# One core, a three-stage kernel: block 0's upper channels moved to ScalarE and GpSimd, ten spare matmuls at the head, and new orders for the first 30 tiles

## The reference

```python
w = exp(weight - max) / (sum + 1e-9)          # 8 heads x 7 taps
x = causal 7-tap convolution of x along S     # one tap set per head of 24 channels
# stage 2, 192 -> 2048 -> 192
h = x @ w_in ;  x = (h * clip(h + 3, 0, 6) / 6) @ w_out
# stage 3, its own weights, rational activation
h = x @ w_in
P = a0 + a1*h + a2*h^2 + a3*h^3 ;  Q = 1 + |b0|*|h| + |b1|*h^2
x = (P / (Q + 1e-6)) @ w_out
```

## Time and profile before

| | us |
|---|---|
| median of 3 runs (1224.21 to 1225.36) | 1225.18 |
| profiled execution | 1226.22 |
| its span, first to last instruction | 1224.4 |
| TensorE busy, 5120 matmuls | 1181.0 (96%) |
| ScalarE busy | 1170.0 (96%) |
| VectorE busy | 1165.9 (95%) |
| GpSimd busy | 1068.5 (87%) |

### The profile page before, as it was taken

How to read it: one execution, slowest core, us unless ns; L and a number is a source line. 1 busy time by engine, 2 the same in 40 slices (tenths; PEclk the granted TensorE clock), 3 DMA queues, 4 the chain that set the end, 5 groups by cost and what they waited for, 6 DMA issues and landing times.

```text
span 1224.4 us, 18261 instructions
## 1 busy us (share of the span) xinstructions
PE 1181.0 (96%) x5120; PEld 962.9 (79%) x5120; DVE 1165.9 (95%) x1792; ACT 1170.0 (96%) x2225; POOL 1068.5 (87%) x828
## 2 busy tenths in 40 slices
PE   4989999999999999999999999999999999999976
PEld 3768888888888888888888888888888888888754
DVE  6879999999999999999999999999999999998897
ACT  5779999999999999999999999999999999999996
POOL 5859989899898999989998998989989899998774
PEclk9999999999999999999999999999999999999998
DMA  4400000000000000010000000000000000000000
GB/s 146 147 1 9 1 23 1 23 9 1 23 1 23 10 23 1 1 31 1 22 1 14 18 1 23 1 23 10 1 23 1 23 1 14 1 1 14 1 14 13
DMA packets 10022, 21.17 MB, mean 17 GB/s; under 512 B 1601, under 2 KB 1857, under 8 KB 9921
## 3 DMA queue, kind: packets, MB, share of 16 engines
q1 hardware_dynamic: 9776, 19.56, 5.4%
q10 hardware_dynamic: 144, 0.46, 0.1%
HBM read 13.72 MB, written 6.29 MB: 16 GB/s over the span
## 4 chain that ended last, share of the span: by engine, by line
PE 83%; DVE 7%; ACT 6%; issue 3%; DMA 0%; POOLq 0%; POOL 0%; ACTq 0%; SPq 0%; DVEq 0%
PE h L263 41%; PE y0b_acc L280 5%; PE y0b_acc L281 4%; PE y0a_acc L275 4%; PE y0a_acc L277 4%; PE y0a_acc L276 4%; PE y1a_acc L275 4%; PE y1a_acc L276 4%; PE y1b_acc L281 4%; PE y1a_acc L277 4%; PE y1b_acc L280 4%; ACT num L353 1%; ACT g_hi L445 1%; ACT rsq L394 1%; DVE num L375 1%
## 5 line engine op out<-in xcount | busy, mean ns | idle before, releaser
L390 POOL TENSOR_TENSOR den<-den,sqr 128x512 f32<-128x512 f32 x248 | 359.8, 1451 | 103.7 <-ACT den L364 103.7
L439 POOL TENSOR_TENSOR g_lo<-g,g_hi 128x512 fp32r<-128x512 f32 x255 | 331.1, 1298 | 3.6 <-ACT g_hi L445 3.6
L346 POOL TENSOR_TENSOR g_lo<-r,g_hi 128x512 fp32r<-128x512 f32 x235 | 308.7, 1313 | 4.2 <-DVE g_lo L346 1.6
L380 DVE SCALAR_TENSOR_TENSOR num<-num,coef,h 128x512 f32<-128x512 f32 x256 | 191.5, 748 | 9.1
L375 DVE TENSOR_TENSOR num<-num,h 128x512 f32<-128x512 f32 x256 | 174.9, 683 | 11.9 <-ACT num L353 5.8
L353 ACT ACTIVATE num<-h,coef 128x512 f32<-128x512 f32 x256 | 181.6, 709 | 0.2
L417 DVE SCALAR_TENSOR_TENSOR h<-num,coef,h 128x512 f32<-128x512 f32 x240 | 179.7, 749 | 0.2
L445 ACT ACTIVATE g_hi<-g 128x512 fp32r<-128x512 f32 x256 | 166.5, 650 | 10.7 <-DVE g L424 2.6
L332 DVE SCALAR_TENSOR_TENSOR r<-r,h 128x512 f32<-128x512 f32 x235 | 160.8, 684 | 8.8 <-ACT r L325 8.0
L394 ACT ACTIVATE rsq<-den 128x512 f32<-128x512 f32 x248 | 158.7, 640 | 7.7 <-POOL den L390 5.0
L410 DVE SCALAR_TENSOR_TENSOR den<-den,h 128x512 f32<-128x512 f32 x240 | 163.2, 680 | 1.1 <-ACT h L406 0.7
(11 more groups left out here) (109 smaller groups left out, 2931.8 us busy)
## 6 DMA issues: line engine op xcount, KB each, us to landing
stage_w<-w_pack SPq DMA_DIRECT2D x15, 448.0 KB, 3.3
raw_a<-x_a SPq DMA_DIRECT2D x16, 259.0 KB, 3.5
out<-y_a SPq DMA_DIRECT2D x16, 256.0 KB, 2.8
out<-y_b SPq DMA_DIRECT2D x16, 128.0 KB, 2.4
...
stage_w<-w_pack ACTq DMA_DIRECT2D x1, 448.0 KB, 3.5
...
tap_ab<-taps SPq DMA_DIRECT2D x1, 7.0 KB, 2.9
```

Source lines behind the costliest of these rows:

```text
L346: eng.tensor_tensor(g1_lo[t % 2][:, :], gated(t)[:, :], f32(g1_hi[t % 2][:, :]), ALU.subtract).then_inc(S["g1lo"], 1)
L380: eng.scalar_tensor_tensor(out=n, in0=n, scalar=a1, in1=h2_of(t), op0=ALU.add, op1=ALU.mult).then_inc(S["num1"], 1)
L390: eng.tensor_tensor(den_of(t), den_of(t), sqr[t % 2][:, :], ALU.add).then_inc(S["den_sum"], 1)
L439: eng.tensor_tensor(g2_lo[t % 2][:, :], g2[t % 2][:, :], f32(g2_hi[t % 2][:, :]), ALU.subtract).then_inc(S["g2lo"], 1)
```

## The change

- **Setup.** The taps and coefs are loaded by ScalarE's queue, raw_a and then chunk 0 by SP's. Abs, Sqrt and its table load come before `w_in_hi(0)`. The second half of the taps is scaled on ScalarE.
- **Block 0's b part.** ScalarE makes seven products (256 wide) in the SBUF tiles num and den, GpSimd adds them in six steps into conv_b. `w_in_lo(1)` moves from GpSimd to VectorE, ahead of `cs_b_lo(0)`.
- **Root.** Its steps stand one by one between the taps of `conv_a`; the register loads move from the setup to pass 3.
- **TensorE** starts with ten matmuls of chunk 0 by itself into a bank that nobody reads then.
- **Plans.** START for passes 0 to 10, a new BEGIN for 11 to 19, RAMP for 20 to 29; MIDDLE from 30 (its only edit takes out an entry that is empty there), END unchanged. W_PACE 1.55. `run` keeps one list of placed steps by block, and `cs_b_hi(0)`, `cs_b_lo(0)` are excluded by it.

```diff
+START = {
+    "sync": [("load_a", AHEAD, 0), ("load_b", PAIR_AHEAD, 9, 0), ("load_w", -4)],
+    "tensor": [("in1", 0), ("out1", 4)],
+    "scalar": [("g1hi", 1), ("w_out_hi", 2), ("w_in_hi", 2), ("relu1", -1), ("conv_a_first", AHEAD, -2),
+             ("registers", 3)],
+    "vector": [("conv_b1", AHEAD, (2, 2, 2, 5, 5, 6, 7), 1), ("gate1", 0),
+             ("conv_a", AHEAD, (1, 5, 5, 7, 8, 11)), ("g1lo", 1)],
+    "gpsimd": [("w_out_lo", 1), ("w_in_lo", 1)],
+}
 BEGIN = {
...
-    "scalar": [("relu1", 0), ("y1a_out", SUM1, 0), ("x2b_hi", SUM1, 0), ("conv_b_first", PAIR_AHEAD, 13, 0),
-             ("g1hi", 1), ("cs_b_hi", AHEAD, 16, 0), ("w_in_hi", 0), ("x2a_hi", SUM1, 0), ("w_out_hi", 1),
-             ("cs_a_hi", AHEAD, 10), ("conv_a_first", AHEAD, 1), ("cs_b_hi", AHEAD, 9, 1)],
...
+    "scalar": [("x2a_hi", SUM1, 1), ("conv_b_first", PAIR_AHEAD, 14, 0), ("cs_b_hi", AHEAD, 3, 1),
+             ("x2b_hi", SUM1, 0), ("relu1", 0), ("y1a_out", SUM1, 0), ("g1hi", 1), ("w_out_hi", 1),
+             ("w_in_hi", 1), ("cs_a_hi", AHEAD, 7)],
+    "vector": [("conv_b_head", PAIR_AHEAD, (16, 17, 17), 0), ("conv_a", AHEAD, (4, 4, 4, 7, 5, 7)),
+             ("gate1", 0), ("g1lo", 1), ("x2b_res", SUM1, -1), ("x2b_lo", SUM1, -1), ("cs_b_lo", AHEAD, -9, 1)],
+    "gpsimd": [("w_out_lo", 2), ("cs_a_lo", AHEAD, 14), ("w_in_lo", 2)],
+}
+RAMP = {
...
+    "tensor": [("in2", 0), ("in1", 0), ("out1", 2), ("out2", 4)],
+    "scalar": [("conv_a_first", AHEAD, -1), ("cs_a_hi", AHEAD, 10), ("w_in_hi", 1), ("rsq2", 1), ("relu1", 0),
+             ("rec2", 1), ("abs2", 0), ("w_out_hi", -2), ("sq2", 0), ("lin2", 0), ("g2hi", 2), ("g1hi", 0)],
+    "vector": [("num2", 1), ("conv_b_tail", AHEAD, (10, 11, 12), 0), ("conv_a", AHEAD, (1, 4, 4, 5, 7, 8)),
+             ("g1lo", 2), ("num1", 1), ("g_neg", 2), ("gate1", 0), ("newton", 1), ("g_first", 1)],
+    "gpsimd": [("x2a_lo", SUM1, -3), ("den_sum", 0), ("w_in_lo", -1), ("w_out_lo", 6), ("g1lo", 0), ("g2lo", 2),
+             ("cs_a_lo", AHEAD, 13)],
 }
-W_PACE = 1.35
+W_PACE = 1.55
+START_END, RAMP_END, END_AT = 11, 30, 258
+WARM = 10
...
+        def product_b(eng, j):
+            if j == 0:
+                eng.wait_ge(d_raw_b0, 32)
+                eng.wait_ge(S["setup_s"], 5)
+            scaled(eng, products[j], raw_b[:, j:j + HALF], tap[1][:, j:j + 1]).then_inc(S["product_b"], 1)
+
+        def add_b(eng, j):
+            eng.wait_ge(S["product_b"], j + 1)
+            if j > 1:
+                eng.wait_ge(S["conv_b_tap"], j)
+            first = products[0] if j == 1 else sums_b(0)
+            eng.tensor_tensor(sums_b(0), first, products[j], ALU.add).then_inc(S["conv_b_tap"], 2 if j == 1 else 1)
...
         @block.tensor
+            eng.wait_ge(S["wi_hi"], 1)
+            for _ in range(WARM):
+                eng.matmul(h1_of(H_BANKS - 1), win_hi[0][:, 0:P], win_hi[0][:, 0:BLK], start=True, stop=True)
...
         @block.scalar
-            load_w(eng, 0)
+            eng.dma_start(tap_ab[:, :], taps[:, :]).then_inc(d_tap, 16)
+            eng.dma_start(coef[:, :], coefs[:, :]).then_inc(d_const, 16)
...
-            w_in_hi(eng, 0)
...
+            w_in_hi(eng, 0)
+            eng.wait_ge(S["setup_v"], TAPS_READY)
+            scaled(eng, tap[1], tap[1], tap_sum[:, 1:2]).then_inc(S["setup_s"], 1)
+            for j in range(K):
+                product_b(eng, j)
+            cs_a_hi(eng, 0)
             w_in_hi(eng, 1)
+            cs_b_hi(eng, 0)
             w_out_hi(eng, 0)
-            cs_a_hi(eng, 0)
...
         @block.vector
             for j in range(K):
                 conv_a_tap(eng, 0, j)
+                if j < 2:
+                    normalize(1, j)
+                else:
+                    eng.wait_ge(*((S["setup_s"], 4) if j == 2 else (S["setup_v"], n_own[0])))
+                    own(refine[j - 2]())
+            eng.wait_ge(S["setup_v"], n_own[0])
+            eng.tensor_tensor(b1_root, s, t, ALU.subtract).then_inc(S["root_done"], 1)
             cs_a_lo(eng, 0)
-            for j in range(K):
-                conv_b_tap(eng, 0, j)
+            w_in_lo(eng, 1)
+            cs_b_lo(eng, 0)
...
         @block.gpsimd
             w_in_lo(eng, 0)
-            w_in_lo(eng, 1)
+            for j in range(1, K):
+                add_b(eng, j)
             w_out_lo(eng, 0)
```

More of the change, by code:

```diff
@@ L36 @@
     "tensor": [("in1", 0), ("out1", 3)],
-    "scalar": [("relu1", 0), ("y1a_out", SUM1, 0), ("x2b_hi", SUM1, 0), ("conv_b_first", PAIR_AHEAD, 13, 0),
-             ("g1hi", 1), ("cs_b_hi", AHEAD, 16, 0), ("w_in_hi", 0), ("x2a_hi", SUM1, 0), ("w_out_hi", 1),
-             ("cs_a_hi", AHEAD, 10), ("conv_a_first", AHEAD, 1), ("cs_b_hi", AHEAD, 9, 1)],
[L40 to L44, removed]
+    "scalar": [("x2a_hi", SUM1, 1), ("conv_b_first", PAIR_AHEAD, 14, 0), ("cs_b_hi", AHEAD, 3, 1),
[6 more added lines that the diff above has]
+RAMP = {
+    "sync": [("load_a", AHEAD, 0), ("load_b", PAIR_AHEAD, 0, 0), ("store_y", SUM2, 1), ("load_w", -4)],
+    "tensor": [("in2", 0), ("in1", 0), ("out1", 2), ("out2", 4)],
[5 more added lines that the diff above has]
+             ("cs_a_lo", AHEAD, 13)],
 }
@@ L504, in y2b_sum @@
                .then_inc(S["y2b_sum"], 1)
+        products = [t[:, i * HALF:(i + 1) * HALF] for t in num + den for i in range(2)][:K]
         def sums_a(k):
@@ L514, in sums_b @@
         def sums_b(k):
[L515 removed]
+            return conv_b[:, :] if k > 1 else conv_b[:, (1 - k) * HALF:(2 - k) * HALF]
         def taps_b(k):
@@ L692, in run @@
                     for i, step in enumerate(steps if isinstance(steps, tuple) else (steps,)):
[L693 to L698, removed]
+                        for k in range(stage in begun, NB):
+                            if (stage, i, k) not in placed and t - lag - step >= k * NF \
+                                    and parity in ([], [k % 2]):
+                                placed.add((stage, i, k))
                                 several[i](eng, k)
@@ L766, in _, with normalize @@
                                   ALU.max, negate=True))
-            normalize(0)
+            total = [tap_sum[:, part:part + 1] for part in range(2)]
+            def normalize(part, step):
+                if step == 0:
+                    eng.wait_ge(S["setup_s"], 1 + part)
+                    own(eng.tensor_scalar(total[part], total[part], 1e-9, None, ALU.add))
+                else:
+                    eng.wait_ge(S["setup_v"], n_own[0])
+                    if step == 1:
+                        own(eng.reciprocal(total[part], total[part]))
+                    else:
+                        own(eng.tensor_scalar(tap[part], tap[part], total[part], None, ALU.mult))
@@ new lines, in _ @@
+            for step in range(3):
+                normalize(0, step)
+            eng.wait_ge(S["setup_v"], n_own[0])
+            s, t, u = root_steps
+            refine = [lambda: eng.tensor_scalar(s, s, 1e-18, None, ALU.max),
+                      lambda: eng.tensor_scalar(t, s, s, b1_abs, ALU.mult, ALU.subtract),
+                      lambda: eng.tensor_scalar(u, s, 2.0, None, ALU.mult),
+                      lambda: eng.reciprocal(u, u),
+                      lambda: eng.tensor_tensor(t, t, u, ALU.mult)]
```

73 lines of the change are left out of this document (34 added, 39 removed).

## The result

The changed kernel takes **1220.49 us** (median of 7, 1220.30 to 1220.87) against 1225.36 (median of 7, 1224.21 to 1226.37) for the kernel before: ratio 0.996, 95% interval 0.9951 to 0.9970, so faster by 0.4%. The forecast was 1219.1. The profiled execution took 1220.49 (before 1226.22), its span 1218.5 (1224.4).

What follows compares the result with a forecast made beforehand. TensorE bounds the kernel, with no idle time in the middle; only the opening, up to about 86 us, can move. -7.1 by in1(20), 0 at pass 20 and +1.0 on GpSimd give -6.1: median 1219.1 us, range 1214.5 to 1223.

Steps and rivals of the forecast that it cites:

- Setup: Opening up to out1(0): coef lands at 4.6, passes 4 and 5 start at 14.9, out1(0) at 19.05; 5.8 us gained.
- rival (c): Opening: coef lands at 6.3 as before, passes 4 and 5 at 16.4, 1.5 less gain, 1220.6; chance 0.04.
- the sign of being wrong: Wrong if passes 4 and 5 start after 16.5, half clock follows out1(0), or in1(20) starts after 62.
- Spare matmuls: Before tile 0: ten, from 6.9 to 11.0, ahead of the first real one at 11.55, so they cost nothing.
- Clock: Full clock behind out1(0), 1.3 us gained there; half clock at pass 20 as before.
- Tiles 1 to 19: From out1(0) to in1(20): a 0.5 stall, 1.0 us of dips, in1(20) at 58.7 against 65.80, -7.1.
- rival (d): Blocks 1 to 3: 16 taps wait for whole GpSimd instructions, 16.8 us more on VectorE, 1233.8; chance 0.04.
- Pass 20: Passes 20 to 23, counted from in1(20) at 58.7: waits shift, half clock as before; sum 0.
- GpSimd's two steps in passes 24 and 25: w_out_lo(14) and (15), 1.15 each, moved there where ScalarE awaits den: +1.0 us, bounds 0 to 2.3.
- Rival (a): Opening gained, not kept: VectorE takes 45.8 us from gate1(0) to gate1(19) again, in1(20) at 62.1, 1222.5; chance 0.20.
- Rival (b): More gain: no dips (1.0), full clock at pass 20 (1.8), GpSimd's steps hidden (1.0): -9.9, 1215.3; chance 0.12.
- The median: Last step of the sum: profiled time 1226.22 becomes 1220.1, and the median is 1.04 lower, 1219.1.

Runs made afterwards that it cites:

- e1: The changed kernel without the ten spare matmuls (WARM 0): 1220.86 us, 0.9965 of the kernel before.
- e5: The changed kernel with block 0's b part back on VectorE, w_in_lo(1) on GpSimd, x0b_hl's split behind the w_out_hi steps: 1222.04 us.
- e7: The changed kernel with win_hi(0) and the products no longer waiting for Abs and Sqrt, the root's steps behind x0b_lo: 1221.79 us.
- e9: e3 with w_in_hi and w_out_hi of BEGIN at lag 2 instead of 0 and 1: 1229.39 us.
- e2: The changed kernel with w_out_lo of chunks 14 and 15 four passes earlier (lag 2 for 6 in RAMP): 1219.28 us.
- e10: e2 with two of the three conv_b1 taps of pass 2 moved to pass 3 in START: 1219.79 us.
- e3: The changed kernel's new setup with the old BEGIN and MIDDLE and W_PACE 1.35: 1226.7 us, 1.0012 of the kernel before.
- e4: The changed kernel's new plans with the old setup, block 0's tap sums back on VectorE, no WARM: 1222.83 us, 0.9982 of the kernel before.

## Why the prediction was right, and where its steps were not

The time fell inside the range with the sign and nearly the size forecast: -5.9 in the span against -6.1. But that it came so near is luck, since its terms missed in both directions. The first matmul of pass 20 came 5.9 us earlier, not 7.1. Passes 20 to 23 gave another 1.8, not 0. Behind pass 24 the kernel lost 2.0, not 1.0, and by the last matmul it had won back 0.3 for which no cause was looked for. (The forecast of 79.9 for pass 24 had the 1.0 in it already, though these steps stand in passes 24 and 25; by its own terms it was 78.9, and measured is 78.34.)

- **Setup: 4.4 gained by out1(0), not 5.8.** The gain of 4.4 is 2.0 of earlier start, 1.1 for five more matmuls behind it and 1.3 of clock. coef was issued at 1.17 as forecast, but took 4.3 us to land, not the 3.4 of before; it is the first link of the changed kernel's chain of waits:

```profile
1.17 4.30 DMA coef<-coefs
```

  ScalarE and GpSimd of the changed kernel:

```profile
5.49 0.20 ACT L790 ACTIVATE beta<-coef 128x2 f32<-128x2 f32 x1 [0.58 <-DMA coef<-coefs]
7.12 0.61 ACT L465 ACTIVATE win_hi<-stage_w 128x512 fp32r<-128x512 f32 x1
8.02 1.71 ACT L586 ACTIVATE num<-raw_b,tap_ab 128x256 f32<-128x256 f32 x4
```

```profile
9.08 0.74 POOL L581 TENSOR_TENSOR conv_b<-num 128x256 f32<-128x256 f32 x1
...
11.71 2.75 POOL L581 TENSOR_TENSOR conv_b<-conv_b,den 128x256 f32<-128x256 f32 x3
```

  Abs to win_hi is 1.63 (1.7 forecast), products are 0.40 apart (0.45), adds 0.88 (0.78). So 0.9 of the 1.4 by which passes 4 and 5 are late is the transfer, the rest the adds. This is rival (c), which had a chance of 0.04: half of its delay of coef came, and nearly all of what it made of it (passes 4 and 5 at 16.27, where it had 16.4 and where 16.5 was the sign of being wrong). Why this small transfer took longer was not tried.
- **x0a_hi at 10.91 (10.85)** is right by two misses. The root's steps between taps cost 0.07 in all, not 0.3; and tap 0 started at 5.32, not 5.0, since the taps landed later.
- **Spare matmuls**: ten in 4.43 us (4.1 forecast), from 7.78 and not 6.9, so they ended at 12.21 and held the first real one by 0.7. The prediction said that each 0.1 of such a delay would show fully. It didn't: x0b_hl came later still, as e1 shows.
- **Clock**: full from tile 0 on, with no pause longer than 1.13 us. Right at out1(0), with e5 as the counter-case; wrong in pass 20, where the clock stayed up behind the split pause: passes 20 to 23 took 18.40 us for their 65 matmuls instead of 20.17.
- **Tiles 1 to 19**: dips of 1.6 to 2.1 in place of 1.5, and a mean of 752 ns for the narrow taps, as in the earlier trace rows. The Trainium skill's rule (SBUF — State Buffer, Who interferes with whom: a VectorE instruction with two SBUF inputs contends with a GpSimd one that reads SBUF) is the one by which rival (d) reckoned. In e7 a step of 0.16 us took 1.18, so such a wait exists. But a narrow tap that ran while GpSimd was idle took 0.48 (e9, at 24.64), so those beside GpSimd's steps waited 0.27 in the mean and not for a whole instruction, and (d)'s 16.8 us didn't come. The prediction also told the page's second sentence short: an instruction with at most one SBUF input is free of this only "outside the 2-port perf modes". The first tap of the group has one tensor as input and took 0.35 us before, 0.63 in the changed kernel and 1.45 in e9, to just behind the end of GpSimd's step beside it; whether it ran in such a mode no run shows.
- **Pass 20**: I walked it with in1(20) first. RAMP lists in2 ahead of in1, so the pass begins with tile 0 of layer 2, for which gate1(19) isn't needed. This was a reading error of the plan, and it hid a miss. VectorE ended gate1(19) at 61.31, not at about 58.6:

```profile
60.61 0.70 DVE L352 SCALAR_TENSOR_TENSOR y1b_acc<-r,h 128x512 f32<-128x512 f32 x1
```

  in1(20) started at 61.79, 3.1 later than forecast and just short of the 62 that was the sign of being wrong. Its wait was filled by the five matmuls of in2(0).
- **GpSimd's two steps in passes 24 and 25**: the bounds were 0 and 2.3, my value 1.0; the offset falls from 7.6 at pass 24 to 5.65 by 202 us, 2.0 us. e2 shows that 1.4 of this is w_out_lo's place. The remaining 0.6 is the pause at x1b_hl before 128.88, which e2 has too and the kernel before hasn't; the sum had no term for it, and its cause wasn't tried.
- **Rival (a)** was stronger than 0.20 says. From the start of gate1(0) to the end of gate1(19) VectorE took 43.6 us, where I had 42.3 and (a) 45.8, and e10 shows it 98% busy ahead of out1's wait. in1(20) came near (a)'s 62.1. The time didn't, because of in2(0) and the clock.
- **Rival (b)'s** 1.8 at pass 20 came, its other parts didn't.
- **The median**: I took 1.04 off the profiled time, as before's profiled execution stood above its median. That execution had a granted clock of 0.993, in the slowest band of the kernel before, and the change takes this loss away: the changed kernel's profiled execution stands on its median (1220.49 both). Of the 1.4 us between forecast and median, this is 1.0.

The setup alone (e3) is 1.3 us slower and the orders alone (e4) 2.5 faster; together 4.9. So half of the gain is the orders' alone, and the setup adds 2.0 to 2.3 under the new orders and takes time under the old ones. The prediction took this for granted by walking the two together. Asking for chunk 3 later is part of what the new orders do, but not enough (e9), and no run splits START, BEGIN and RAMP, so which of their entries make the earlier tile 0 pay stays open.
